# Token grams as 64x64 products, a score mask on another engine, and a new order of the head

## The reference

```python
# 1 attention with the delta rule, per batch (2) and head (8), head width 48, 768 steps
y[t]   = q[t] @ state
v_old  = k_n[t] @ state                      # k_n is k divided by its norm
state += beta[t] * outer(k_n[t], v[t] - v_old)
# 2 MLP
h    = x @ w_in                              # 384 -> 1024
solu = h * softmax(h)
x2   = normalized(solu) * g_ln @ w_out       # 1024 -> 384
# 3 mixture of 8 experts, top 1, capacity 384
out[i] = gate * relu(x2[i] @ w1[e]) @ w2[e]
```

## Time and profile before

| | |
|---|---|
| three executions | 481.85, 482.38, 482.74 us |
| the profiled execution, as timed | 482.99 us |
| its span, first to last instruction | 481.1 us |
| TensorE matmuls busy | 401.4 us (83%), 5935 of them |
| VectorE, ScalarE, GpSimd busy | 302.2, 217.6, 79.2 us |
| mean granted TensorE clock | 0.938 |
| first solve of group 0 | 61.46 us |
| first MLP matmul of group 0 | 100.45 us |
| routing begins | 290.15 us |

### The profile page before, as it was taken

How to read it: one execution, slowest core, us unless ns; L and a number is a source line. 1 busy time by engine, 2 the same in 40 slices (tenths; PEclk the granted TensorE clock), 3 DMA queues, 4 the chain that set the end, 5 groups by cost and what they waited for, 6 DMA issues and landing times. The chain is left out here.

```text
span 481.1 us, 13925 instructions
## 1 busy us (share of the span) xinstructions
PE 401.4 (83%) x5935; PEld 378.6 (79%) x5936; DVE 302.2 (63%) x557; ACT 217.6 (45%) x389; POOL 79.2 (16%) x77
## 2 busy tenths in 40 slices
PE   2356689599999979999979990469999999899992
PEld 2355688488999858999868990459999999899992
DVE  4899458649946769963423627548568668555660
ACT  1333621137752115772114745037676776556650
POOL 3400200000060000050000000270423423401112
PEclk9999999769999989999979996569999999999997
DMA  6796100328510069000041018624475485362000
GB/s 134 260 199 182 26 3 4 69 65 196 216 37 19 5 127 203 18 34 21 4 96 38 16 35 299 240 72 159 153 290 178 161 288 198 131 227 70 19 7 23
DMA packets 27815, 54.39 MB, mean 113 GB/s; under 512 B 4404, under 2 KB 21360, under 8 KB 27280
## 3 DMA queue, kind: packets, MB, share of 16 engines
q1 hardware_dynamic: 23648, 48.04, 33.5%
q0 software_dynamic: 3072, 4.73, 3.2%
q10 hardware_dynamic: 1040, 0.79, 0.7%
HBM read 44.11 MB, written 9.44 MB: 111 GB/s over the span
## 5 line engine op out<-in xcount | busy, mean ns | idle before, releaser
L1341 PE MATMUL PS<-xTh,w1h 128*128 128x256 f32 (+1 forms) x192 | 56.8, 296 | 3.5 <-DVE xTl L1261 1.8
L1342 PE MATMUL PS<-xTl,w1h 128*128 128x256 f32 (+1 forms) x192 | 56.2, 293 | 0.0
L1343 PE MATMUL PS<-xTh,w1l 128*128 128x256 f32 (+1 forms) x192 | 56.2, 293 | 0.0
L967 PE MATMUL PS<-w_in_h,mlpT 128*128 128x512 f32 x144 | 50.9, 430 | 4.0 <-DMA mlpT<-yT 4.0
L1287 POOL DMA_INDIRECT xd<-x,giu x24 | 28.6, 1190 | 108.2 <-DVE giu L1244 95.2
L1341 PE MATMUL PS<-w2h,hTh 128*128 128x384 f32 x136 | 46.1, 339 | 0.0
L1343 PE MATMUL PS<-w2h,hTl 128*128 128x384 f32 x136 | 45.5, 335 | 0.0
L1342 PE MATMUL PS<-w2l,hTh 128*128 128x384 f32 x136 | 45.5, 334 | 0.0
L1267 DVE SCALAR_TENSOR_TENSOR hTl<-PS,hTh 128x384 fp32r<-128x384 f32 x64 | 35.5, 554 | 12.9 <-ACT hTh L1127 10.5
L1341 PEld LDWEIGHTS PS<-xTh,w1h 128*128 128x128 f32 x192 | 37.4, 195 | 4.5 <-issue 2.1
L1294 POOL DMA_INDIRECT out<-yo,oiu x24 | 24.2, 1008 | 100.2 <-ACT yo L1138 75.0
(11 more groups left out here) (167 smaller groups left out, 891.6 us busy)
## 6 DMA issues: line engine op xcount, KB each, us to landing
w1r<-w SPq DMA_DIRECT2D x8, 1536.0 KB, 6.3
w2r<-w SPq DMA_DIRECT2D x8, 1536.0 KB, 10.4
KP<-kv SPq DMA_DIRECT2D x3, 1536.0 KB, 12.0
mlpT<-yT SPq DMA_DIRECT2D x12, 288.0 KB, 4.1
QT<-qt SPq DMA_DIRECT2D x6, 384.0 KB, 6.4
out<-zero SPq DMA_DIRECT2D x12, 192.0 KB, 4.0
x<-rowst SPq DMA_DIRECT2D x12, 192.0 KB, 1.9
yT<-w_out_t SPq DMA_DIRECT2D x1, 1536.0 KB, 6.4
```

The costliest lines, as they stand in the source:

```text
L967: last = pe.matmul(PS[:, h_bank(n) + s, :], mlpT[:, n, x, c, :], w[:, c, o], start=(c == 0 and j == 0), stop=(c == KD - 1 and j == 2))
L1341: pe.matmul(out_ap, lhs[0], rhs[0], start=first, stop=False)
L1342: pe.matmul(out_ap, lhs[0], rhs[1], start=False, stop=False)
L1343: return pe.matmul(out_ap, lhs[1], rhs[0], start=False, stop=final)
```

## The change

1. `grams` becomes 64 products of 64x64 a group (one for each chunk, pair and parity). The diagonal block of an odd block of tokens now lies in columns 32 to 63. A new ScalarE step, `odd_blocks`, copies it to columns 0 to 31 of the same PSUM rows, ahead of the transpose in `systems`. In group 0 ScalarE copies one of the two and VectorE the other. `kk` rises four times a group.
2. The score mask moves from GpSimd to VectorE. In group 0 ScalarE still copies, and VectorE multiplies all of it by a 0/1 tile `later_c` in one instruction (`mask_first`), after its first `solution`. In groups 1 and 2 `take_scores` goes, and VectorE multiplies straight from PSUM, in two halves inside the MLP.
3. TensorE's `grams(1)` goes ahead of `fold`.
4. The four weight loads for the fold are issued by ScalarE, after `take_scores(0)`; `w_out_t` lands in `XE`. SP's queue goes on with `load_kt(1)`, `load_kv(0)`, `w_in` and the keys of group 2, with no wait for the fold between them.
5. The split of `w_in` leaves the fold and stands in ScalarE's `attention(0)`, after the two solutions. `systems(1)` on VectorE comes after the split of `w_out`; `solution(0, 1)` comes ahead of `scales(1)`.

The core of the diff:

```diff
-                sp.wait_ge(kk, 8)
-                sp.dma_start(w_out_t_sb, ...)
-                sp.dma_start(wg[:], ...)
-                sp.dma_start(gl[:], g_ln)
-                sp.dma_start(w_raw[:, :, 0:DM], ...)
+                sp.wait_ge(kk, 4)
                 load_kt(1)
                 load_kv(0)
-                sp.wait_ge(wfold, 1)
                 sp.dma_start(w_in_raw, ...)
...
+                def odd_blocks(g):
+                    act.wait_ge(kk, 4 * (g + 1))
+                    for c in range(1 if g == 0 else 2):
+                        b = block(2 * c + 1)
+                        last = act.activation(grams_at(g)[b, :, 0:BL], grams_at(g)[b, :, BL:CH], ACT.Copy)
+                    last.then_inc(a_od, 1)
...
                 first_kt(act, 1)
+                odd_blocks(0)
                 gram_blocks(0)
                 take_scores(0)
+                act.dma_start(w_out_t_sb, ...)
+                act.dma_start(wg[:], ...)
+                act.dma_start(gl[:], g_ln)
+                act.dma_start(w_raw[:, :, 0:DM], ...)
+                odd_blocks(1)
                 fold()
...
                 def systems(g):
-                    dve.wait_ge(kk, 8 * (g + 1))
+                    dve.wait_ge(kk, 4 * (g + 1))
+                    dve.wait_ge(a_od, g + 1)
+                    if g == 0:
+                        link(dve.tensor_copy(grams_at(0)[block(3), :, 0:BL], grams_at(0)[block(3), :, BL:CH]))
...
+                def mask_first():
+                    dve.wait_ge(e_pt, 1)
+                    dve.tensor_tensor(PT, PT, later_c[:, :].unsqueeze(1).to_broadcast([P, NU, CH]), ALU.mult).then_inc(masked, 2)
+                def mask_scores(g, par):
+                    dve.wait_ge(qk, 4 * (g + 1))
+                    dve.wait_ge(uy, 2 * NC * g)
+                    dve.tensor_tensor(PT[:, HP * par:HP * par + HP], scores_at(g, par), later_c[:, :]..., ALU.mult).then_inc(masked, 1)
...
-                        for q in range(P // BL):
+                        for c in range(2):
                             for par in range(2):
-                                o = chunk(q // 2) if q % 2 == 0 else block(q)
-                                w = CH if q % 2 == 0 else BL
-                                last = pe.matmul(grams_at(g)[block(q), HP * par + i, 0:w], KT[g % 2][half(par), i, block(q)], KT[g % 2][half(par), i, o], start=True, stop=True)
+                                tokens = KT[g % 2][half(par), i, chunk(c)]
+                                last = pe.matmul(grams_at(g)[chunk(c), HP * par + i], tokens, tokens, start=True, stop=True)
...
                 grams(0)
                 scores(0)
+                grams(1)
                 fold()
-                grams(1)
                 between(0)
```

More of the change, by code:

```diff
@@ L71, in build @@
         later = sb("later", [P, P])
+        later_c = sb("later_c", [P, CH])
         zero = sb("zero", [P, DM])
@@ L106, in build @@
         dve_step, root_done, low_ready, t_ready, td_ready, v_scaled, e_as, e_pt, z_tt, d_tt, d_x, e_gt, e_qe, d_s, e_yl = sems("dve_step root_done low_ready t_ready td_ready v_scaled e_as e_pt z_tt d_tt d_x e_gt e_qe d_s e_yl")
-        e_gx, e_tb, e_m1, e_tt, a_x, a_s, e_yh = sems("e_gx e_tb e_m1 e_tt a_x a_s e_yh")
+        e_gx, e_tb, e_m1, e_tt, a_x, a_s, e_yh, a_od = sems("e_gx e_tb e_m1 e_tt a_x a_s e_yh a_od")
         nmax, e_exp, p_mul, p_ctr, p_var, e_ltr, e_llo, e_x2 = sems("nmax e_exp p_mul p_ctr p_var e_ltr e_llo e_x2")
@@ L308, in _ @@
                 pool.affine_select(out=later[:], in_=ones[:], compare_op=ALU.is_gt, fill=0.0, base=0, pattern=[[1, P]], channel_multiplier=-1).then_inc(const_ready, 1)
+                pool.affine_select(out=later_c[:], in_=ones[:, 0:CH], compare_op=ALU.is_gt, fill=0.0, base=0, pattern=[[1, CH]], channel_multiplier=-1).then_inc(const_ready, 1)
                 pool.memset(zero[:], 0.0).then_inc(zero_ready, 1)
@@ L330, in strictly_lower @@
                     pool.affine_select(out=Ts, in_=As[:], compare_op=ALU.is_gt, fill=0.0, base=0, pattern=[[1, BL], [-1, BL]], channel_multiplier=0).then_inc(below, 1)
[L332 to L337, removed]
                 strictly_lower(0)
-                later_only(0)
                 pool.wait_ge(consts2, 4)
+                pool.wait_ge(below, 1)
                 clear_t(0)
@@ L484, in mlp @@
                     mlp_var(g, 2)
-                    if ahead:
-                        take_scores(g + 1)
                     mlp_ln(g, 2, 1)
@@ L517, in _ @@
                 first_kt(act, 1)
+                odd_blocks(0)
                 gram_blocks(0)
                 take_scores(0)
+                act.dma_start(w_out_t_sb, w_out_t.rearrange("(c p) f -> p c f", p=P)).then_inc(ld_wt, 16)
+                act.dma_start(wg[:], w_gate.rearrange("(c p) e -> p c e", p=P)).then_inc(ld_wt, 16)
+                act.dma_start(gl[:], g_ln).then_inc(ld_wt, 16)
+                act.dma_start(w_raw[:, :, 0:DM], w_out.rearrange("(k p) n -> p k n", p=P)).then_inc(ld_wt, 16)
+                odd_blocks(1)
                 fold()
@@ L636, in attention @@
                         scales(g + 1)
-                    solution(g, 1)
+                    if g:
+                        solution(g, 1)
                     if ahead:
@@ L690, in _ @@
                 dve.memset(St[:], 0.0).then_inc(s_clear, 1)
-                dve.wait_ge(const_ready, 4)
+                dve.wait_ge(const_ready, 5)
                 for par in range(2):
-                    last = dve.tensor_copy(eye2[half(par)], ident[half(par), half(par)])
+                    dve.tensor_copy(eye2[half(par)], ident[half(par), half(par)])
+                last = dve.tensor_copy(later_c[chunk(1)], later[chunk(1), chunk(1)])
                 last.then_inc(s_clear, 1)
@@ L711, in _ @@
                 scale_v(0)
-                systems(1)
                 dve.wait_ge(w_hi, 1)
                 dve.tensor_tensor(w_out_l[:], w_raw, w_out_h[:].bitcast(F32), ALU.subtract).then_inc(w_lo, 1)
+                systems(1)
                 lower_block(0)
+                solution(0, 1)
+                mask_first()
                 for g in range(GROUPS):
@@ L742, in _ @@
                     mlp_lo(g, 2, 0)
+                    if ahead:
+                        mask_scores(g + 1, 0)
                     mlp_lo(g, 2, 1)
```

22 lines of the change are left out of this document (11 added, 11 removed).

## The result

The changed kernel takes 484.66 us (median of 20 runs, 480.67 to 487.68); the kernel before, on the same chip, 481.69 us (median of 20, 478.28 to 484.72). The ratio is 1.0063, with a 95% interval of 1.0039 to 1.0087: slower by 3.0 us. The forecast was 483.9, within 477.5 to 487.0.

The account below looks back on a forecast made before the run. TensorE was taken as the bound, idle in the head for weights and at instruction-block waits. Terms +1.7 (first solve), +2.9 (mask) and -3.05 (grams of group 2) gave +1.55: 483.9 us against the median, range 477.5 to 487.0.

Parts of the forecast that it names:

- F: Start of TensorE's `fold` in the head, 29.61 us before; forecast 40, as its weights share the DMA engines with other loads.
- the bounds 30 to 42.1: Range for the fold's start in us: 30 if ScalarE's queue is served first, 42.1 if it is served last.
- From F to S (23.2): Head, fold's start to first solve: fold, `w_out` scale and split, `lower_rows`, `between`'s copy, `lower_block`, summing to 23.2 us.
- S: Start of the first solve on TensorE, 61.46 us before; forecast 63.2, a cost of +1.7 us.
- the sentence behind it on what leaves the path: Head: 5 us leave the fold's tail (2.8 split, 2.2 ScalarE waiting), some 9 us of grams leave the path.
- The mask in group 0 (+2.9): VectorE's mask, 2.2 us, and later steps delay `gate` and `step_matrix` after the first solve: +2.9 us, lowest +2.3, highest 3.5.
- Groups 1 and 2: Mask on VectorE in the MLP, where TensorE is the bound: no cost, 0 to +0.5 us.
- Grams of group 2 (-3.05): Attention: grams done 2.1 us after their start, instruction wait moves to the output step, clock falls, MLP starts 3.05 us earlier.
- G: Start of the grams of group 2 on TensorE, 85.50 us before; the wait was forecast to end 6 us after it.
- The rival in which the clock holds: Attention, output steps: clock stays up, grams term -6.9 us, sum -2.3, 480.0 us; chance 0.25.
- +1.55: Forecast sum of all terms, +1.7, +2.9 and -3.05 us, on 482.99: slower, 484.5 us for the profiled execution.
- a fold before 36: Head: if `fold` starts before 36 us, the prediction of a slower kernel is wrong on its sign.

Follow-up runs that it names:

- Holding `w_in` alone: Changed kernel with `w_in` and the keys of group 2 held on SP until the fold's four loads landed: 474.24 us, ratio 0.9857.
- holding `kv` too: Changed kernel with `kv`, `w_in` and the keys of group 2 held on SP until the fold's four loads landed: 472.76 us, ratio 0.9829.
- The early mask: Changed kernel with VectorE's group 0 mask moved from behind `solution(0, 1)` to right behind `scale_v(0)`: 482.19 us, ratio 1.0019.
- the mask alone: Kernel before with only the score mask moved from GpSimd to VectorE, in all groups: 485.21 us, ratio 1.0082.
- the new grams alone: Kernel before with only the 64x64 grams and the moved odd blocks: 471.54 us, ratio 0.9808.
- the old grams: Changed kernel with the grams of before (products of 32 tokens, no moved blocks): 492.34 us, ratio 1.0225.
- the loads sooner: Changed kernel with `kv` and all behind held, VectorE reordered and ScalarE's four load issues moved ahead, behind its first block copy: 468.66 us, ratio 0.9737.
- the weights first: Changed kernel with the fold's four loads issued by SP, ahead of keys 1, `kv`, `w_in` and keys 2, nothing held: 473.73 us, ratio 0.9853.

## Why the prediction was right, and where it was not

**The weights (F = 40).** Measured 40.93, inside the bounds 30 to 42.1. The reasoning holds: the sum of all loads that start together, at the observed share, with the weights near the end. Holding `w_in` alone moves F to 31.63 and holding `kv` too to 26.75, so the competing loads are shown to be the cause. The choice of 40 between these bounds was a judgement, not a sum. One detail was wrong. I had ScalarE issue from 17.3 to 20.6, behind `take_scores(0)`; its queue issued from 14.62 to 16.6, while the activation ahead in its order still ran (ScalarE, after; ACTq is its queue):

```profile
14.62 0.41 ACTq L519 DMA_DIRECT2D XE<-w_out_t  x1
16.14 0.46 ACTq L522 DMA_DIRECT2D QG<-w_out  x1
```

It cost the forecast nothing, since the backlog decides and not the issue. The Trainium skill, DMA: Bandwidth & Descriptors, section on queues, rings and completion order, says that an engine takes turns between queues by whole packets; q10, with 1984 packets beside 1123 of q1, did end last, and F = 40.93 is nearer to 42.1 than to 30. That agrees, but it does not test the rule: a queue that is simply served last would end the same way, and whether the packets of the profile are those of the page no run here shows.

**From F to S (23.2).** Measured 64.14 - 40.93 = 23.21, and 23.21 in the kernel with `w_in` held as well; before it was 31.85. The sum of the steps was right, but the sentence behind it on what leaves the path was not. In before, ScalarE waited for `w_in` for 5.63 us and not 2.2 (ScalarE, before):

```profile
49.97 2.77 ACT L515 ACTIVATE w_in_h<-yT 128x3072 fp32r<-128x3072 f32 x1 [5.63 <-DMA yT<-w_in]
```

Wait and split make 8.4 of the 8.6 us that the way from F to S is shorter. The 9 us of `grams(1)` ran beside them and left no path of their own.

S moved by +2.68 instead of +1.7; the difference is that F came 0.93 later than 40.

**The mask in group 0 (+2.9).** `gate` at S + 8.13 (S + 8.6 forecast), `step_matrix` at S + 10.57 (S + 11.15): +2.28, at the lowest bound of that term. The early mask gave 2.5 us back, the mask alone cost 3.4. Groups 1 and 2 cost nothing that can be seen, as forecast. The factor chain ended at 40.4 instead of 46.1 (41 to 42.5 forecast). The Trainium skill, SBUF — State Buffer, section Who interferes with whom, has a VectorE instruction with two inputs in SBUF contend with a GpSimd instruction that reads SBUF; the trace agrees: the step takes 2.78 us in before and 2.75 with the new grams alone, where GpSimd's mask runs, and 0.96 in after and with the mask alone, where it does not.

**Grams of group 2 (-3.05).** The grams were done within G + 2.2, the wait moved to the output step, and the clock fell to 0.50, all as forecast. The wait was 2.42 us instead of 3.8, because the block arrived at G + 4.7 and not G + 6. The first MLP matmul came at G + 10.07 instead of G + 11.9: -4.88 us. The gain was undersized by 1.8: 1.3 because of the arrival, and 0.5 because what follows it took 5.37 us and not 5.9. I had taken the arrival as G + 6 because the transfers of `mlpT` are the same, and they do lie at the same place (SyncE issues them 1.2 us ahead of G in before and 1.0 in after). Yet the block arrives at G + 4.90, 5.97 and 7.05 with the old grams (mask alone, before, old grams), and at G + 4.15 to 5.24 with the new ones, where a wait shows. With the loads sooner none shows. So the step that was wrong is to hold the arrival fixed; what sets it stays open. The rival in which the clock holds did not come: 2.42 us of idleness too were followed by 0.50.

**Not foreseen: +0.84 us of clock.** VectorE's mask makes TensorE wait 2.04 us ahead of `gate`, and 6 us later its granted clock is 0.50 for 3.3 us (the window 78.40 to 81.70 above). The stretch from `step_matrix` to G took 16.59 us, before 15.75. The second `gate` call (L868, 62 matmuls) tells it in one row, first in after, then in the kernel with the mask early:

```profile
79.08 3.01 PE L868 MATMUL PS<-KP,XE 64*48 64x112 f32 x62
```

```profile
77.66 1.70 PE L868 MATMUL PS<-KP,XE 64*48 64x112 f32 x62
```

The same 2 us of waiting are followed by a fall in before with the mask alone (3.20 us for these 62) and in the kernel with `kv` and all behind held. It is absent from the traces with the mask early, where the wait is not there either. With the weights first the wait is 1.97 us, the granted clock was 0.50 up to 60 us, and it is the first `gate` call that is slow (3.23 us for 64). But with `w_in` held, and with old grams, the wait is there (2.04 and 2.05 us) and the 62 take 1.70. So the wait alone does not decide it, and what does stays open.

**The sum.** At the first MLP matmul the terms give 2.68 + 2.28 + 0.84 - 4.88 = +0.92 us (101.37 against 100.45), where the forecast has +1.55. That it is so near is in part luck: the terms missed by +0.98 (F), -0.62 (mask), +0.84 (clock) and -1.83 (grams).

The spans differ by 2.1, and the forecast expected nothing behind the first MLP matmul. From there to the first solve of group 1 it is +0.94 (46.99 us against 46.05). The new grams alone show the same (47.01), so it is not the mask. The granted clock stays at 0.50 for 4.3 us of the MLP in after and for 3.5 in before, which makes some 0.4 of it, an estimate; the rest is open.

Behind that, the two kernels take the same: 334.8 us to the end in after, 334.6 in before. Within this stretch the falls of the clock lie differently. After is 2.3 us quicker up to the first TensorE matmul of the routing, and 2.5 slower from there to the end, where no line has changed. The windows, before first, then two of after (columns as above):

```profile
247.30:254.10 6.80, 6.20 (x21) 4.83 (x22) 0.69 (x1) 0.60 (x1) 0.00 (x0) 0.50 0.44 98
```

```profile
249.00:252.40 3.40, 3.26 (x8) 2.58 (x9) 0.12 (x1) 0.00 (x0) 0.00 (x0) 0.50 0.54 112
412.90:416.20 3.30, 3.30 (x12) 3.30 (x11) 1.02 (x2) 0.90 (x2) 2.69 (x3) 0.50 0.20 53
```

The fall near 249 us is half as long as in before, and there is a further one about 122 us behind the start of the routing. Four of the twelve kernels show both (after, after with the mask early, after with old grams, before with the mask alone). They take 142.3 to 143.2 us from the first solve of group 1 to the routing and 191.9 to 192.7 from there to the end; the other eight take 143.7 to 145.4 and 189.4 to 190.75. Over all twelve the two stretches together take 333.0 to 336.0 us. So a single profile carries up to 3 us that belong to no part of the change, and a stretch that looks slower can be paid for by the one ahead of it. The medians decide: +3.0 us. The traces show 2.1 of it; before's profiled execution was 1.0 us further above its median than after's, which covers the rest. The +3.0 is twice the +1.55 forecast.

**What the prediction missed although its number held.** I costed the new grams by what they do to TensorE and took the later loads as given. In before's order they release SyncE's loads 4.4 us earlier, and alone they are worth 10.0 us, with 6.1 of them already there at S. With the mask at +3.4, the queues and the order must have cost about 9.6, if the parts add (-10.0 + 3.4 + 9.6 = +3.0); the change of order alone was not run. Holding loads back gives a like amount, -10.4 and -11.9 against after. I wrote that 9 us of grams are "spent on a fold that starts 10 us later". Against what the grams alone allow, it starts 16.6 us later (40.93 against 24.35). The number held because S was worked out as a whole, from the landing of the weights on, and not as a sum of gains and losses. The sentence on which its sign hung, that a fold before 36 would turn it round, was right: each variant of the changed kernel with such a fold is faster than before.

## What to carry to other kernels

Look at which instruction releases each load: shortening the work ahead of it starts the later loads earlier, and the gain may be larger than the work saved. A second DMA queue brought little here, where the engines were already busy for 0.92 of the time (235 GB/s before, 251 with two queues at 0.95). It took from the transfer that TensorE waited for, so hold back what nobody waits for, and put the consumers in the order in which the data comes. An operation moved to an engine is priced by what stands behind it in that place: in the changed kernel the mask of 2.28 us cost 2.5 us more behind the first `solution` than where VectorE was idle.

## What the runs showed of the hardware that I had not expected

A load's issue can block its queue for long: 7.09 us for `w_in` in after, 15.78 with the weights first, against 0.39 in before, and the loads behind it wait too. Why it takes so long no run tests; each time much had been issued ahead of it (SyncE's queue, after):

```profile
11.96 7.09 SPq L273 DMA_DIRECT2D yT<-w_in  x1
19.16 1.77 SPq L240 DMA_DIRECT2D KT<-kt  x2
```

In the kernel with the weights first, the record of the granted clock begins earlier and shows 0.50 for most of the head. Its windows:

```profile
5.20:12.20 7.00, 4.91 (x210) 4.73 (x213) 3.93 (x7) 2.27 (x2) 0.00 (x0) 1.00 0.77 177
12.40:60.00 47.60, 27.70 (x546) 27.16 (x540) 35.30 (x49) 21.59 (x32) 4.42 (x4) 0.50 0.60 156
```

Its scores (10.98 to 13.61) took 2.63 us for 128 matmuls, partly at 1.00, where after's took 3.69. After's head is shown as 1.00 without a record, although its scores run at the slower rate. At a recorded 1.00 the 126 gram matmuls of the same shape, at 91.38, took 2.08 us. So in the head the duration of a known matmul is the better witness of the clock.

The wait between blocks of instructions is not a fixed price: 3.20 to 5.42 us inside grams of 32-token products, which use up a block sooner, and 1.60 to 2.53 in or behind grams of 64x64 products, where one shows at all. Identical code took from 189.4 to 192.7 us from the routing to the end, from one profile to the next.
